# Two first up parts woven, two rows of a tap scaled on ScalarE, and a last addition done by stacked identities

## The reference

```python
w = np.exp(weight_gen - max); w = w / (sum(w) + 1e-9)      # (2, 4096, 8 heads, 7 taps)
x1[b, s, h] = sum over k of w[b, s, h, k] * x_pad[b, s + k, h]   # tap 6 is the token itself
h = x1 @ moe_w_in;   x2 = np.maximum(0.01 * h, h) @ moe_w_out
h = x2 @ moe2_w_in;  out = np.where(h > 0, h, np.exp(np.minimum(h, 0)) - 1) @ moe2_w_out
```

## Time and profile before

| | us |
|---|---|
| median of 3 runs (lowest, highest) | 1130.13 (1129.84, 1130.41) |
| profiled execution, its own time | 1129.72 |
| its span | 1127.9 |
| TensorE busy in the span | 1119.7 (99%) |
| ScalarE, VectorE, GpSimd busy | 744.0, 624.5, 390.4 |
| granted clock of TensorE over the span | 0.999 |

### The profile page before, as it was taken

One profiled execution on the slowest core, in us unless ns is written; L12 is line 12 of the kernel. 1 busy time (PEld: TensorE's weight loads), 2 busy tenths in 40 slices (PEclk: granted clock), 3 DMA queues, 4 the chain that ended last, 5 costly groups with the idle time before them and its releaser, 6 DMA issues.

```text
span 1127.9 us, 22691 instructions
## 1 busy us (share of the span) xinstructions
PE 1119.7 (99%) x9794; PEld 921.8 (82%) x9794; DVE 624.5 (55%) x654; ACT 744.0 (66%) x837; POOL 390.4 (35%) x407
## 2 busy tenths in 40 slices
PE   8999999999999999999999999999999999999998
PEld 6888888888888888888888888888888888888886
DVE  8677547365463645636456364554736546363555
ACT  6577657576575766757567575765757657576676
POOL 6663622607135080440805317062260713500000
PEclk9999999999999999999999999999999999999999
DMA  5412020211202102021020201102021120110001
GB/s 173 119 50 85 17 81 15 82 29 29 82 1 82 29 28 83 1 82 29 29 82 3 88 22 57 54 19 83 11 82 29 29 82 2 43 29 29 15 1 57
DMA packets 46080, 54.88 MB, mean 49 GB/s; under 512 B 4254, under 2 KB 34718, under 8 KB 45980
## 3 DMA queue, kind: packets, MB, share of 16 engines
q1 hardware_dynamic: 45836, 53.30, 15.6%
q10 hardware_dynamic: 144, 0.11, 0.0%
HBM read 35.71 MB, written 17.69 MB: 47 GB/s over the span
## 4 chain that ended last, share of the span: by engine, by line
PE 98%; DVE 1%; ACT 0%; DMA 0%; issue 0%; DVEq 0%
PE y_a L730 31%; PE hidden L609 31%; PE y_b L713 21%; PE hidden L614 10%; PE hidden L665 5%; DMA wk<-in_weight_gen_dram 0%; PE hidden L699 0%; DVE prod L1233 0%; DVE act L1233 0%; PE y_b L856 0%; DVE mix L1233 0%; PE hidden L666 0%; DVE staged L1233 0%; DVE act L1236 0%; DVE raw_d L1233 0%
## 5 line engine op out<-in xcount | busy, mean ns | idle before, releaser
L730 PE MATMUL y_a<-hid_hi,dn 64*128 64x512 f32 x2048 | 625.5, 386 | 0.0
L730 PEld LDWEIGHTS y_a<-hid_hi,dn 64*128 64x128 f32 x2048 | 375.7, 184 | 40.0
L713 PE MATMUL y_b<-hid_hi,dn 64*128 64x512 f32 x1024 | 395.5, 386 | 0.0
L713 PE MATMUL y_b<-hid_lo,dn 64*128 64x512 f32 x1024 | 395.4, 386 | 0.0
L730 PE MATMUL y_a<-hid_lo,dn 64*128 64x512 f32 x1024 | 394.4, 386 | 0.0
L609 PE MATMUL hidden<-in_a_hi,up_a_hi 64*128 64x512 f32 x1016 | 294.1, 387 | 0.2
L609 PE MATMUL hidden<-in_a_lo,up_a_hi 64*128 64x512 f32 x1016 | 293.6, 386 | 0.0
L609 PE MATMUL hidden<-in_a_hi,up_a_lo 64*128 64x512 f32 x1016 | 293.6, 386 | 0.0
L614 PE MATMUL hidden<-in_b,up_b_hi 64*128 64x512 f32 x1016 | 293.6, 386 | 0.0
L1380 DVE TENSOR_TENSOR hid_lo<-hidden,hid_hi 128x1024 fp32r<-128x1024 f32 x124 | 151.6, 1222 | 255.0 <-ACT hid_hi L1109 255.0
L1380 DVE TENSOR_TENSOR hid_lo<-act,hid_hi 128x1024 fp32r<-128x1024 f32 x131 | 165.5, 1264 | 189.2 <-ACT hid_hi L1109 189.2
(11 more groups left out here) (143 smaller groups left out, 1312.3 us busy)
## 6 DMA issues: line engine op xcount, KB each, us to landing
xw<-in_x_dram SPq DMA_DIRECT2D x14, 960.0 KB, 5.2
raw_b<-squares_out SPq DMA_DIRECT2D x60, 96.0 KB, 2.2
out_dram<-staged SPq DMA_DIRECT2D x15, 384.0 KB, 2.6
squares_in<-prod SPq DMA_DIRECT2D x56, 96.0 KB, 2.0
squares_out<-ya SPq DMA_DIRECT2D x15, 256.0 KB, 2.0
raw_a<-squares_in SPq DMA_DIRECT2D x14, 256.0 KB, 2.9
raw_d<-in_moe_w_out_dram SPq DMA_DIRECT2D x8, 384.0 KB, 3.4
squares_out<-yb SPq DMA_DIRECT2D x15, 128.0 KB, 2.2
```

The lines of the kernel that those rows point to most:

```text
L713: return nc.tensor.matmul(y_b[d // ST % 2][:, :], dn[m][rows, f, P:2 * P], v[rows, s % HB, HALF[i]], start=start, stop=stop)
L730: return nc.tensor.matmul(y_a[bank][:, :], dn[m][rows, f, w:w + P], v[rows, s % HB, HALF[i]], start=start, stop=stop)
```

## The change

1. SyncE loads both first weight chunks (`wk[0]`, `wk[1]`); the second was ScalarE's first instruction.
2. Product 6 on VectorE covers two of the four rows. ScalarE scales the other two (`scale_row`): for each row 8 copies of 24 columns with a scale for each partition. `prod` becomes the fourth term in FIRST_TERMS.
3. `up_first_two` weaves the up parts of steps 0 and 1: four products of step 1 stand between step 0's low products and its 64-feature products, the rest of step 1 behind step 0. Step 1's `up_pair` comes after the first half of up part 2.
4. ScalarE rounds the third quarter (`round_up(0, 2)`) before step 0's leaky part, not after its rounding.
5. At phase 1, down part 6 is opened before up part 8, and closed between its two halves. The second half of down part 7's close moves between the two halves of up part 10.
6. At the end ScalarE copies all 128 rows of `y_b` in two halves of 256 columns (`last_b`). TensorE multiplies them by `halves_sum`, 128 x 64, two 64 x 64 identities one above the other, which turns and adds at once. GpSimd makes `halves_sum` after its last mix.

```diff
+        last_b = raw_a[:, 0:T]
+        halves_sum = soft0[:, :, :].rearrange("p a k -> p (a k)")[:, 0:D2]
...
+        s_scaled = sem("newest_tap_rows_scaled")
...
         s_outt = sem("out_transposed")
+        s_lastb = sem("last_y_b_halves_copied")
+        s_halves = sem("stacked_identity_ready")
...
-        FIRST_TERMS = ((prod, 1), (prod2, 3), (mix, 4), (staged_rows, 5), (term4, 11))
+        FIRST_TERMS = ((prod2, 3), (mix, 4), (staged_rows, 5), (prod, 1), (term4, 11))
+        SCALED_ROWS = J // 2
...
             load_w(0)
+            load_w(1)
             sp.dma_start(xw[:, PAD:, :], x_rows[:, 0:J * D].rearrange("p (j d) -> p j d", d=D)).then_inc(s_x0, 16)
...
+            nc.gpsimd.tensor_tensor(halves_sum, ident[:, 0:D2], ident[:, D2:P], ALU.add).then_inc(s_halves, 1)
...
-            def up_first():
-
-                def product(i, w, v, **flags):
-                    return nc.tensor.matmul(hidden[:, 0, HALF[i]], w[0][:, i * P:(i + 1) * P], v[input_of(0, 0)][:, :], **flags)
-
+            def up_first_two():
+                src = input_of(0, 0)
+
+                def product(s, i, w, v, **flags):
+                    cols = slice((2 * s + i) * P, (2 * s + i + 1) * P)
+                    return nc.tensor.matmul(hidden[:, s, HALF[i]], w[0][:, cols], v[src][:, :], **flags)
+
+                def a_hi(s):
+                    for i in (0, 1):
+                        product(s, i, up_a_hi, in_a_hi, start=True, stop=False)
+                        product(s, i, up_a_lo, in_a_hi, start=False, stop=False)
+
+                def a_lo(s):
+                    for i in (0, 1):
+                        product(s, i, up_a_hi, in_a_lo, start=False, stop=False)
                 pe.wait_ge(s_xhi, 1)
                 pe.wait_ge(s_uplo, 1)
-                for i in (0, 1):
-                    product(i, up_a_hi, in_a_hi, start=True, stop=False)
-                    product(i, up_a_lo, in_a_hi, start=False, stop=False)
-
+                a_hi(0)
                 pe.wait_ge(s_xin, 1)
-                product(0, up_a_hi, in_a_lo, start=False, stop=False)
-                product(1, up_a_hi, in_a_lo, start=False, stop=False)
+                a_lo(0)
+                a_hi(1)
                 pe.wait_ge(s_uphi, 2)
                 pe.wait_ge(s_xin, 2)
-                product(0, up_b_hi, in_b, start=False, stop=False)
-                product(1, up_b_hi, in_b, start=False, stop=False)
+                for i in (0, 1):
+                    product(0, i, up_b_hi, in_b, start=False, stop=False)
                 pe.wait_ge(s_uplo, 2)
                 pe.wait_ge(s_xup, 1)
-                low, high = up_pair(0, input_of(0, 0), 0, stop=True)
+                low, high = up_pair(0, src, 0, stop=True)
                 low.then_inc(s_up1, 1)
                 high.then_inc(s_up, 1)
-
-            def up_whole(m, src, s):
-
-                def product(i, w, v, **flags):
-                    cols = slice((2 * s + i) * P, (2 * s + i + 1) * P)
-                    return nc.tensor.matmul(hidden[:, s % 2, HALF[i]], w[m][:, cols], v[src][:, :], **flags)
-
-                up_pair(m, src, s, start=True)
-                for i in (0, 1):
-                    product(i, up_a_hi, in_a_hi, start=False, stop=False)
-                    product(i, up_a_lo, in_a_hi, start=False, stop=False)
-                    product(i, up_a_hi, in_a_lo, start=False, stop=False)
-                    product(i, up_b_hi, in_b, start=False, stop=True).then_inc(s_up if i else s_open, 1)
+                a_lo(1)
+                product(1, 0, up_b_hi, in_b, start=False, stop=False)
+                product(1, 1, up_b_hi, in_b, start=False, stop=False).then_inc(s_open, 1)
...
                 down_a(m, s, d, HIGH, 1, 2)
-            def down_close(m, s, d):
-
-                down_a(m, s, d, LOW, 0, 2)
-                pe.wait_ge(s_ybfirst, d + 1)
-                down_b(m, s, d, HIGH, 0, 0)
-                down_a(m, s, d, LOW, 1, 0)
-                down_b(m, s, d, HIGH, 0, 1)
+            def down_close(m, s, d, halves=(0, 1)):
+
+                if 0 in halves:
+                    down_a(m, s, d, LOW, 0, 2)
+                    pe.wait_ge(s_ybfirst, d + 1)
+                    down_b(m, s, d, HIGH, 0, 0)
+                    down_a(m, s, d, LOW, 1, 0)
+                    down_b(m, s, d, HIGH, 0, 1)
...
                     pe.wait_ge(s_termv, steps - end)
+                    if term is prod:
+                        pe.wait_ge(s_scaled, SCALED_ROWS)
                     for j in range(J):
...
+                pe.wait_ge(s_halves, 1)
+
                 def turn_a(j):
                     nc.tensor.transpose(out_bank[j][:, 0:P], ya[:, j * P:(j + 1) * P], ident[:, :])
                 def turn_b(j):
-                    nc.tensor.transpose(out_bank[j][:, P:D], yb[1][:, j * P:(j + 1) * P], ident[0:D2, 0:D2]).then_inc(s_outt, 1)
+                    nc.tensor.matmul(out_bank[j][:, P:D], last_b[:, j * P:(j + 1) * P], halves_sum, start=True, stop=True).then_inc(s_outt, 1)
                 for h in (0, 1):
                     pe.wait_ge(s_ya, CH + h)
                     turn_a(2 * h)
                     turn_a(2 * h + 1)
-                    pe.wait_ge(s_yb, LAST + 1 + h)
+                    pe.wait_ge(s_lastb, 1 + h)
                     turn_b(2 * h)
                     turn_b(2 * h + 1)
             def phase(m, c, ph, dm, dc):
                 for s in range(ST):
                     g = ST * ph + s
-                    if known(ph) and g == 0:
-                        up_first()
+                    if g == 0:
+                        up_first_two()
+                    if g < 2:
                         continue
...
                         pe.wait_ge(*down_split(0, DN_PARTS - 1))
-                        down_alone(0, ST - 2, g - 2)
+                        pe.wait_ge(s_lo, g - 1)
+                        down_open(0, ST - 2, g - 2)
+                        down_middle_apart(0, ST - 2, g - 2)
                     if s == 0:
...
                         pe.wait_ge(s_g, ST * c_two + (s - 2) % ST + 1)
-                    if ph == 0 and s == 1:
-                        up_whole(m, input_of(m, c), s)
-                        continue
                     up(m, input_of(m, c), g, s, False)
+                    if g == 2:
+
+                        up_pair(0, input_of(0, 0), 1, stop=True)[1].then_inc(s_up, 1)
+                    if (ph, s) == (1, 0):
+                        down_close(0, ST - 2, g - 2)
+                    if (ph, s) == (1, 2):
+                        down_close(0, ST - 1, g - 3, (1,))
                     if (ph, s) in ((0, 2), (1, 0), (1, 2)):
                         up(m, input_of(m, c), g, s, True)
                         continue
...
+                    down_close(of, step, d, (0,) if (ph, s) == (1, 1) else (0, 1))
             sum_first_mix()
...
                     nc.scalar.activation(last_columns(ya[:, :], True), last_columns(y_a[1 - ph % 2][:, :], False), ACT.Copy).then_inc(s_ya1, 1)
-                    copy_low()
+
+                    act_e.wait_ge(s_dn, END + 1)
+                    b, b0 = last_columns(last_b, True), last_columns(y_b[ph % 2][:, :], False)
+                    for js in (slice(0, J // 2), slice(J // 2, J)):
+                        nc.scalar.activation(b[:, :, js], b0[:, :, js], ACT.Copy).then_inc(s_lastb, 1)
                     return
...
                 rounding(0, 0, 0, 0)
-                round_up(0, 2)
...
                         if (ph, s) in DN2_AT:
                             round_down(1, DN2_AT.index((ph, s)))
-            act_e.dma_start(wk[1][:, :, :], w_rows[:, J * H * TAPS:2 * J * H * TAPS].rearrange("p (a k) -> p a k", k=TAPS)).then_inc(s_w[1], 16)
             softmax_exp(0)
             softmax_exp(1)
+            def scale_row(j):
+
+                for h in range(H):
+                    cols = slice(h * GROUP, (h + 1) * GROUP)
+                    last = nc.scalar.activation(prod[:, j, cols], xw[:, PAD + j, cols], ACT.Copy, scale=soft0[:, j * H + h, PAD:PAD + 1])
+                last.then_inc(s_scaled, 1)
+
+            act_e.wait_ge(s_x0, 16)
+            act_e.wait_ge(s_soft0, FIRST_SOFT_STEPS)
             for n, (term, steps) in enumerate(FIRST_TERMS[:-1]):
+                if n < SCALED_ROWS:
+                    scale_row(n)
+                if term is prod:
+                    act_e.wait_ge(s_scaled, SCALED_ROWS)
                 act_e.wait_ge(s_termv, steps)
                 nc.scalar.activation(packed[n].rearrange("p (j d) -> p j d", j=J), term[:, :, P:D], ACT.Copy).then_inc(s_pack, 1)
...
             round_down(0, 0)
+            round_up(0, 2)
...
                 dve.wait_ge(s_soft0, FIRST_SOFT_STEPS)
-                product(6, prod, 0, J)
+                product(6, prod, SCALED_ROWS, J)
...
                 a, a0 = last_columns(ya[:, :], True), last_columns(y_a[LAST % 2][:, :], False)
```

(9 more changed lines are left out.)

3 lines of the change are left out of this document (2 added, 1 removed).

## The result

The changed kernel takes 1131.37 us in the median of 22 runs (1130.70 to 1132.84), the kernel before, beside it, 1129.95 (22 runs, 1129.68 to 1131.56). The ratio is 1.0013, 95% interval 1.0007 to 1.0018: 1.4 us slower, where 0.45 faster was forecast, and outside the range given. The runs of before lie together but for one. Those of the changed kernel fall apart: ten at 1130.70 to 1131.03, nine at 1131.3 to 1132.2, three at 1132.7 to 1132.84. The profiled execution is one of the lower group: 1130.75, span 1129.0 (before: 1129.72 and 1127.9).

A forecast was written before the change was run, and what follows sets the result against it. Outside TensorE's full middle, the first 37 us were taken as bound by a VectorE-ScalarE-VectorE chain. Start +0.1, turn 0.0 and -0.3, end -0.25 sum to -0.45: 1129.3 us profiled, 1129.7 median; range 1128.9 to 1130.7.

The forecast's parts named there:

- The middle can't change: From 62 to 1105 us TensorE is busy throughout, so the change acts only before 62 and after 1122.7.
- the 0.21 at which it would have been waited for: Start, ScalarE's row scaling: 0.15 us per instruction taken; at 0.21 the packed mix's slack of 0.4 is gone.
- the chain: Start: step 0's leaky part at 19.65 leads through ScalarE and TensorE to step 2's leaky part at 24.55, against 24.46.
- The pause at 59.5: Turn into phase 1: TensorE's wait before up part 10's second half, to be filled by down part 7; -0.3 us.
- each record costs 0.112: Start, TensorE's mix groups: every record takes 0.112 us, with the first group starting at 7.65 instead of 6.93.
- 1.34 a group of twelve: Start, TensorE: a mix group of twelve records takes 1.34 us; four groups end at 13.1.
- the transfers ahead of it are the same, and they drained just before; I take 19.1: Start: the third quarter's last piece, issued at 14.85, lands at 19.1; bounds 18.2 to 19.6.
- the upper bound of +0.6: Start of step 2's leaky part: forecast +0.1 us, bounds -0.35 and +0.6, the latter with the quarter landing at 19.6.
- The second rival: Start: the quarter lands late, and ScalarE, with step 0's leaky part behind it, holds TensorE; +0.55, 1130.7 us; chance 0.15.
- two costs at their upper ends: Needed for 1130.7 us: 4.7 us landing and 0.25 us scaling instructions, putting the quarter's landing at 20.1.
- Its pause goes in full: -0.3: Turn into phase 1: up part 10 starts 0.45 earlier, at 57.7, and its pause at 59.5 vanishes; -0.3 us.
- I take -0.25: End: SyncE's last output issue comes at 1125.2 to 1125.4 against 1125.57; -0.25 us, bounds -0.4 and 0.

The follow-up runs named there:

- after_up2_late: The changed kernel with the split of MLP 2's second quarter of up weights moved from step 1 to step 2 of phase 1; 1131.30 us.
- no_scale_front: no_scale with the third quarter's rounding ahead of step 0's leaky part; 1132.26 us, ratio 1.0016 to the kernel before.
- after_warm: The changed kernel with one more product on zeros (256 columns) ahead of the first mix group; 1131.61 us.
- end_delayed: end_only with a memset of 0.48 us ahead of VectorE's first copy of the last outputs; 1129.98 us.
- end_only: The kernel before with the change's new end alone; 1130.42 us, ratio 1.0003.
- no_scale_b: The same program as no_scale, timed again; 1129.64 us.
- no_scale: no_end without ScalarE's scaled rows: VectorE makes product 6 whole and its group is first on TensorE again; 1129.55 us.
- no_end: The changed kernel with the third quarter's rounding back in its old place and the old end; median 1131.01 us.
- warm2_up2: no_end with two more products on zeros ahead of the first mix group and the up-weight split a step later; 1129.11 us.
- after_round_back: The changed kernel with the third quarter's rounding back behind the rounding of step 0; 1130.05 us.
- weave_only: The kernel before with the two first up parts woven and nothing else; 1130.08 us, ratio 1.0000.

## Why the prediction was wrong

**Right.** The middle can't change. VectorE is sooner in the mix (last term 12.73, 13.19 before; forecast 0.33 sooner, it was 0.46, as the first weight chunk landed sooner). Scaling takes 0.2 a copy (eight in 1.75), not 0.15, still under the 0.21 at which it would have been waited for. The first group is issued at 7.61. From a given start of step 0's leaky part the chain holds to a tenth: I had 19.65 to 24.55, the trace has 20.04 to 24.96. The pause at 59.5 goes.

**Wrong, the start.** Two steps failed. "each record costs 0.112" and "1.34 a group of twelve": the first group took twice that, since I moved TensorE's first work 0.7 us back (the newest term to fourth place) and counted this as a start time only. I had the pause in hand, 0.86 in the earlier trace rows, and did not ask what a longer one does. In some executions it costs nothing, in others 1.0 to 1.1 us of the mix (the inputs of the first up part at 15.67 and 15.84, against 14.70). The second is "the transfers ahead of it are the same, and they drained just before; I take 19.1", with bounds of 18.2 and 19.6. The issue-to-landing time of the quarter was read once, in one execution and at one issue time, and taken to move with the issue. For its 256 KB piece it was 5.0 to 6.4 in the seventeen traces that issue it at 12.3 to 13.4, and 3.4 in the two that issue it at 14.8 and 14.9; an issue at 12.35 landed no sooner than one at 13.1. The last piece, for which I took 19.1, came at 19.6, 19.8 and 20.6 where ScalarE waited for it (after_up2_late, no_scale_front, after_warm), and step 2's leaky part started 0.72, 0.87 and 2.84 later than before: past the upper bound of +0.6. The second rival had the mechanism, place and sign, at a chance of 0.15, and I held against it that it needed two costs at their upper ends. The late landing alone was enough, and the rival did not count the half pace that follows TensorE's wait.

**Wrong, phase 1.** "Its pause goes in full: -0.3": it went, and up part 12 then waited for the rest of step 10 at 65.17. ScalarE is back to back from step 9 to step 10, with the two copies of a split of weights between; I followed the gain to up part 10 and its one operand, and not on to the next place where TensorE meets that chain.

**Wrong, the end.** The last issue comes 0.35 sooner in relation to the last down part (forecast 0.25). The step that failed stands nowhere in words: "I take -0.25" is worked out up to SyncE's last issue, and the time from there to the end of the span was taken to stay at 2.33. It was 3.26: 0.9 us of landing against 0.35 of gain. What goes with it in every trace of the new end but end_delayed's is a fetch of instructions among the last stores, which it has 1.6 to 2.0 after the first store's issue and the old end 0.2 to 0.5. Why the new end moves it there is open, and so is whether the fetch is the whole cause: no run moved the fetch alone.

The sum by measured parts, from medians: new end +0.54 (end_only), the quarter ahead +2.6 at full pace of the mix (no_scale_front less no_scale_b; by the profiles only 1.8 of this is the start, the rest a fetch beside the last stores), the rest -0.25 to -0.35 (no_scale), the clock in the mix 0 to +1.5 (no_end). They don't add up to the +1.4 of the whole, and need not: at half pace the mix is later and the quarter, issued at 14.77, landed in 3.4 us with nothing waiting for it, so the two exclude each other in part. Which of the causes makes an upper run of the changed kernel is not shown. It was profiled in its lower group only, and the mean clock does not part its groups: 0.998 to 1.0 in the lower ten, 0.997 to 1.0 in the nine above them, 0.997 or 0.998 in the top three. A late quarter, as in after_warm's profile (1132.98), a lost clock and a fetch of q8 are all candidates.

Versions with a lower median than both: no_scale (woven parts, weight chunk on SyncE, new down parts; old end, no scaling, the quarter in its old place) at 1129.55 and 1129.64, with the split moved 1129.30, and warm2_up2, which has the scaled rows and their two products on zeros as well, at 1129.11, against 1129.86 to 1129.90. For the last the ratio is 0.9992 [0.9983, 1.0001], which still holds 1, but its highest run (1129.33) is below the lowest of before (1129.70); its 0.75 us is the sum of leads that the trace shows, and its last sum of y_a starts at 1122.01, 1122.75 before.

## What to carry to other kernels

Before a copy of freshly loaded data is moved ahead of a step that others wait for, take the landing from several executions and price the queue behind it, the pace that a waiting TensorE loses included. Reordering that lets TensorE start later must be charged for its clock, not only for the shift; a product on zeros in the gap is cheap. Follow a removed pause to the next place where the same two engines meet. A shorter path to the last store's issue is not yet a shorter kernel: when the time from the issue to the end grows, look at what else the DMA engines carry beside the last stores. And when a delay put in as a test makes the kernel faster, compare where everything else went before blaming the time: the test may have moved that too.

## What the runs showed of the hardware

- TensorE's pace after a pause differs from run to run: full after 1.55 us without work (after_round_back) and after 1.63 (weave_only), half after 1.54 (the changed kernel), granted clock 0.50 after 2.44 (no_end) and after 2.42 (after_warm). The clock column did not show the loss in the changed kernel.
- The 256 KB of the quarter took 5.0 to 6.4 us to land when issued at 12.3 to 13.4, and 3.4 when issued at 14.8 and 14.9.
- Instruction fetches use the DMA engines at the end of the kernel. Where one falls among the last stores, the time from the last issue to the end is 3.1 to 3.9 us, and 2.3 to 2.5 where none does. Where the q14 fetch falls changes with the program of the end.
- A second small load (112 KB) on another queue, issued beside the first, delayed the first by 0.44 us (VectorE's first reduction at 3.22, against 2.78 and 2.79).
